# A two-layer feed-forward kernel with Winograd-style products: the next tile's x is split at the tile border, and one output block is carried in a PSUM bank

## The chip, the cores and the metric

The kernel runs on one core of a Trainium2 chip. The metric is the device time of one execution in microseconds (us). Before the change it is 1216.26 us, the median of three runs (1216.18 to 1216.88).

## The reference

An attention over 4 batches, 8 heads and 768 positions of width 64 (chunks of 32 queries that see 16 keys to the left, 8 to the right and 8 memory keys) gives a matrix of 3072 tokens by 512. Two feed-forward layers follow:

```
x = attention(q, k, v, mem_k, mem_v)            # 3072 x 512
h = x @ w_in;   g = where(h > 0, h, exp(min(h, 0)) - 1);   x = g @ w_out      # 512 -> 2048 -> 512
h = x @ w_in2;  g = s * max(h, 0)**2 + b;                  out = g @ w_out2   # 512 -> 2048 -> 512
```

All of it is float32. The kernel reaches the precision by writing every operand of a product as a high part and a low part.

## The kernel before, in words

**Tiles and products.** The 3072 tokens are cut into three tiles of 1024. Layer 0 takes them as tiles t=0, 1, 2, layer 1 as t=3, 4, 5 (the fourth to the sixth tile). A 2x2 block product is made with seven products instead of eight, in the order P1, P5, P6, P2, P7, P4, P3; blocks are called 11, 12, 21, 22. The sums of blocks that the products need are made beforehand: of x by GpSimd (`sums_of_x`, lines 806 to 816), of the weights by GpSimd (`prepare`), of g by VectorE (`sum_of`, line 1437).

**Steps.** TensorE's work is a list of 672 steps of six matmuls of 512 columns, 112 steps to a tile. Within a tile, s=0 to 27 is the up part of group 0 (two rounds of seven products by two steps), s=28 to 55 the down part of group 0 (seven products by four steps), s=56 to 69 and 70 to 83 the two up rounds of group 1, and s=84 to 111 the down part of group 1. A down product has four steps; x, the place within a down part, runs from 0 to 27, so that P1 is x=0 to 3, P7 x=16 to 19, P4 x=20 to 23, P3 x=24 to 27. `up` (line 989) multiplies with xc_hi and xc_lo, `down` (line 1004) with g_hi and g_lo. Steps and t count from 0.

**Banks.** Six accumulators of PSUM are in use: `acc_a` (P1, P2, P4), `acc_g` (P5, P3), `acc_e` (P6, P7), two banks each. `wait_bank` (line 958) is where TensorE waits for a bank: for P1 until the last block 21 is read out (`c21_done`), for P4 until block 11 is read out of `acc_a`. ScalarE seeds `acc_e` with P1's sum (`seed`, line 1132) and copies it out twice (`copy_s2`, line 1138, after P6; `copy_s3`, line 1144, after P7).

**The output y.** Group 0 writes the four blocks of y; group 1 adds to them. Block 21 in group 1 takes two additions of VectorE: `add_y21_u3` (after P7, at x=20 and 21) and `add_y21_p4` (after P4, at x=24 and 25), both by `add` (line 1354).

**Splits.** For each down step ScalarE makes g_hi (`cut_g`, line 1202) three steps ahead and VectorE g_lo (`lo_g`, line 1442) one iteration later; their ring has four places. For the next tile's x, ScalarE makes xc_hi (`split_x`, line 1122) and VectorE xc_lo (`lo_x`, line 1347) one iteration later: 14 pairs of 128x512 elements, one for each product and each kk in 0, 1. Which step makes which is the table `SPLIT_AT` for t=1 and 2 (it has kk=1 at s=107, 108, 110, 111, 113, 115 and 117) and `SPLIT_LATE` for t=3, 4, 5. The sums of x for kk=1 are made in place, so that GpSimd waits in `sums_of_x` until the low parts of P1 and later P2 are made.

**Weights.** GpSimd and ScalarE prepare the weights of both layers during the products: 7 pieces for each of 32 sets m. For a piece, ScalarE makes the high part (`cut_w`, line 1216) at the step that `hi_slot` names, GpSimd the low part (line 774), and SyncE's queue saves it to DRAM (line 617, 256 KB), from four places in turn (`wait_w_free`: a place is free when its save has landed). SyncE's queue also loads the weights of two steps at a time (line 636, 512 KB) into a ring of four. The 56 pieces of m=24 to 31 (layer 1, group 1) are made from t=2, s=94 on to t=3, s=70.

**Order.** There is no scheduler: ScalarE and VectorE each go through one loop over g, the number of the step, and emit in a fixed order within it what the tables place there. ScalarE: seeds and copies, then `relu` or `exp`, then `cut_g`, `split_x`, `cut_w`, then pieces of attention or copies of the output. VectorE: additions of the up part, P3's additions, `elu_of` or `square_of`, `sum_of`, `lo_g`, additions to y, `lo_x`, attention. GpSimd's order is written out at lines 834 to 858. In t=4 and 5 TensorE transposes the output of the tile before (`transpose_out`, line 955) ahead of every second step from s=2 to s=16; the first of them waits for both of P3's additions (`c12_done`).

Of the kernel before, what the change touches and what calls it, by code (L numbers as in the profile page):

```python
# [10 lines left out]
ACT = mybir.ActivationFunctionType  # L11
# [23 lines left out]
HALF = 512  # L35
TOK = 2 * HALF
TPL = NTOK // TOK
TILES = 2 * TPL
QUADS = 4
PHASE = 7 * QUADS  # L40
GROUP = 2 * PHASE
PER_TILE = 2 * GROUP
STEPS = PER_TILE * TILES
P1, P5, P6, P2, P7, P4, P3 = range(7)
X11, X12, X21, X22 = range(4)
# [120 lines left out]
def copies_before(r):  # L166
    return 2 * (r - r // 6)
# [36 lines left out]
def hi_slot(pp):  # L204

    if pp < PRODUCTS:
        return 4 + (pp - HEAD_PREP) * 11 // 10 + (3 if pp >= PREP_AT[PAIR + 1, P1] else 0)
    if pp < WIDE_END:
        return PER_TILE + 4 + (pp - PRODUCTS) * 3
    if pp < WIDE_END + 28:  # L210
        return 2 * PER_TILE + 2 + (pp - WIDE_END) * 5 // 2
    return 2 * PER_TILE + 94 + (pp - WIDE_END - 28) * 8 // 5


HI_SLOT = {pp: hi_slot(pp) for pp in range(HEAD_PREP, 2 * PRODUCTS)}
# [6 lines left out]
def saves_due(d):  # L222
# [6 lines left out]
HEAD_ORDER = [(c, pi) for c, pi, _ in HEAD_SPLITS]  # L229
SPLIT_AT = ((92, 93, 95, 96, 97, 98, 100), (107, 108, 110, 111, 113, 115, 117))  # L230
LOAD_AT = (88, 102)
SPLIT_LATE = ((P1, 0, 73), (P1, 1, 75), (P5, 0, 77), (P5, 1, 80), (P6, 0, 87), (P6, 1, 89), (P2, 0, 93), (P2, 1, 95),
              (P7, 0, 101), (P7, 1, 103), (P4, 0, 113), (P4, 1, 114), (P3, 0, 115), (P3, 1, 116))
LATE = [(pi, kk) for pi, kk, _ in SPLIT_LATE]
OUT_BLOCKS = TOK // 128
# [52 lines left out]
def build(nc, q, k, v, mem_k, mem_v, w_in0, w_out0, w_in1, w_out1, s_in, b_in, out):  # L288
# [8 lines left out]
    with ctx:  # L297
# [3 lines left out]
        def sem(name):  # L301
            return ctx.enter_context(nc.semaphore(name))
# [143 lines left out]
        c21_done = sem("c21_done")  # L446
        c12_done = sem("c12_done")
        y12_u2 = sem("y12_u2")
        y21_u3 = sem("y21_u3")
        y22_u3 = sem("y22_u3")  # L450
        y11_copied = sem("y11_copied")
        y11_added = sem("y11_added")
# [281 lines left out]
        def _(pool):  # L734
# [111 lines left out]
                sums_of_x(2, kk)  # L846
            for m in range(SETS + 4, SETS + 8):
                prepare((m,))
            for kk in range(2):
                sums_of_x(3, kk)  # L850
            for m in range(SETS + 8, 2 * SETS - 2):
                prepare((m,))
            sums_of_x(4, 0)
            for m in range(2 * SETS - 2, 2 * SETS):
                prepare((m,))
            sums_of_x(4, 1)
            for kk in range(2):
                sums_of_x(5, kk)

        @block.tensor  # L860
        def _(pe):
# [96 lines left out]
            def wait_bank(st, i):  # L958
                r = st.round
                if st.pi == P1 and r:  # L960
                    pe.wait_ge(c21_done, 2 * (r - 1) + i + 1)
                elif st.pi == P5 and r:
                    pe.wait_ge(c12_done, 2 * (r - 1) + i + 1)
                elif st.pi == P6:
                    pe.wait_ge(seeded, 2 * r + i + 1)
                elif st.pi == P7:
                    if r % 6 == 5:
                        pe.wait_ge(y12_u2, 2 * st.t + i + 1)
                    else:
                        pe.wait_ge(s2_done, copies_before(r) + i + 1)  # L970
                elif st.pi == P4:
                    wait_c11_read(pe, r, i)
                elif st.pi == P3:
                    pe.wait_ge(c22_done, 2 * r + i + 1)
# [20 lines left out]
            def down(st):  # L995
                k = split_of(st)
                pe.wait_ge(g_lo_done, k + 1)
                w = w_ring[:, st.g // 2 % W_RING, st.g % 2]
                for d in range(2):
                    if st.i == 0:  # L1000
                        wait_bank(st, d)
                    cols = slice(128 * d, 128 * d + 128)
                    for n, (a, x) in enumerate(((0, g_hi), (1, g_hi), (0, g_lo))):
                        last = nc.tensor.matmul(bank_of(st.pi, d), w[:, a, cols], x[:, k % RING, :],  # L1004
                                                start=(st.pi in (P1, P5, P4) and st.i == 0 and n == 0),
                                                stop=(st.i == QUADS - 1 and n == 2),
                                                skip_group_check=True)
                last.then_inc(step_done, 1)
# [61 lines left out]
        def _(act):  # L1070
# [53 lines left out]
            def seed(r, i, after):  # L1124
                act.wait_ge(step_done, after + 1)
                if r == 0:
                    act.wait_ge(e_cleared, i + 1)
                if r and r % 6 == 0:
                    act.wait_ge(y22_u3, 2 * (r // 6 - 1) + i + 1)
                elif r:  # L1130
                    act.wait_ge(s3_done, copies_before(r - 1) + i + 1)
                nc.scalar.activation(acc_e[i][:, :], acc_a[i][:, :], ACT.Copy).then_inc(seeded, 1)  # L1132

            def copy_s2(r, i, after):
# [11 lines left out]
            def copy_y11(p, d):  # L1146
                act.wait_ge(step_done, p.start + QUADS * P2 + QUADS)
                wait_y_free(act, p.t)
                nc.scalar.activation(y[:, d, 0:HALF], acc_a[d][:, :], ACT.Copy).then_inc(y11_copied, 1)

            def relu_of(d, pi, i):
                m = item_of(d.t, d.gr, 2 * d.u + i, pi)
# [90 lines left out]
            for g in range(STEPS + 2):  # L1243
# [10 lines left out]
                for p, x in downs_at(g):  # L1254
                    for d in range(2):
                        if x == 4 + d:
                            seed(p.round, d, p.start + QUADS * P1 + 3)
                        if x == 12 + d and p.gr == 0:
                            copy_s2(p.round, d, p.start + QUADS * P6 + 3)
                        if x == 16 + d and p.gr == 0:  # L1260
                            copy_y11(p, d)
                        if x == 20 + d and p.gr == 0:
                            copy_s3(p.round, d, p.start + QUADS * P7 + 3)
                for d, pi, i in items_at(g, 0):
                    if d.t >= TPL and pi == C11:
# [35 lines left out]
        def _(dve):  # L1301
# [48 lines left out]
            def y_at(b, d):  # L1350
                return y[:, d + 2 * (b // 2), HALF * (b % 2):HALF * (b % 2) + HALF]

            def add(to, a, b, done):
                nc.vector.tensor_tensor(to, a, b, ALU.add).then_inc(done, 1)  # L1354

            def make_c22(r, i, to, t=None):
                dve.wait_ge(s3_done, copies_before(r) + i + 1)
                if t is not None:
                    wait_y_free(dve, t)
                add(to, s3[:, i, :], acc_g[i][:, :], c22_done)  # L1360
# [22 lines left out]
                dve.wait_ge(y11_copied, 2 * p.t + d + 1)  # L1383
                add(y_at(X11, d), y_at(X11, d), acc_a[d][:, :], y11_added)

            def add_y21_u3(p, d):
                dve.wait_ge(step_done, p.start + QUADS * P7 + 4)
                dve.wait_ge(c21_done, 2 * (p.round - 3) + d + 1)
                add(y_at(X21, d), y_at(X21, d), acc_e[d][:, :], y21_u3)

            def add_y22_u3(p, d):
                dve.wait_ge(step_done, p.start + QUADS * P7 + 4)
                dve.wait_ge(c22_done, 2 * p.round + d + 1)
                add(y_at(X22, d), y_at(X22, d), acc_e[d][:, :], y22_u3)

            def add_y21_p4(p, d):
                dve.wait_ge(step_done, p.start + QUADS * P4 + 4)
                dve.wait_ge(y21_u3, 2 * p.t + d + 1)
                add(y_at(X21, d), y_at(X21, d), acc_a[d][:, :], c21_done)

            def add_y12_p3(p, d):
                dve.wait_ge(step_done, p.start + QUADS * P3 + 4)
# [64 lines left out]
            for g in range(STEPS + 2):  # L1467
# [26 lines left out]
                for p, x in downs_at(g):  # L1494
                    for d in range(2):
# [5 lines left out]
                        else:  # L1501
# [3 lines left out]
                                add_y12_u2(p, d)  # L1505
                            if x == 16 + d:
                                add_y11(p, d)
                            if x == 20 + d:
                                add_y21_u3(p, d)
                            if x == 22 + d:  # L1510
                                add_y22_u3(p, d)
                            if x == 24 + d:
                                add_y21_p4(p, d)
                for xt, kk, pi in x_split_at(g - 1):
                    lo_x(xt, kk, pi)
                for n, at in woven_at(g):
# [33 lines left out]
```

## Time and profile before

| | |
|---|---|
| median of 3 runs | 1216.26 us |
| profiled execution, its own time | 1211.64 us |
| its span, from the first to the last instruction | 1209.9 us |
| mean granted TensorE clock, as a share of full speed | 0.975 |
| busy: TensorE, VectorE, ScalarE, GpSimd | 1116.7, 845.4, 757.0, 425.8 us |
| attention before the first step, about | 120 us |
| bytes moved by DMA | 302.80 MB |

The profile names engines PE (TensorE's matmuls), PEld (its weight loads), DVE (VectorE), ACT (ScalarE), POOL (GpSimd) and SPq (SyncE's queue). A row of instructions has the source line, the engine, the operation, the tile written and the tiles read, the shapes and the count; behind the bar stand the busy time in us, the mean duration of one in ns, and the idle time of the engine ahead of them with what ended most of it. An instruction's duration reaches into the next one: VectorE's additions of 0.68 us start 0.60 us apart. Times of steps in the text are the starts of a step's first matmul.

### The profile page before, as it was taken

How to read it: one execution, taken by the hardware profiler on the slowest of the kernel's cores; microseconds unless marked ns; L12 is line 12 of the kernel's file. 1: busy time of each engine (PE TensorE's matmuls, PEld its weight loads, DVE VectorE, ACT ScalarE, POOL GpSimd, SP SyncE). 2: the span in 40 equal slices, each digit the busy share in tenths (PEclk: the TensorE clock that was granted, in tenths of full speed). 3: DMA queues.
4: the chain of work that ended last, by engine and by line, in shares of the span. 5: the costliest groups of instructions: out<-in, count | busy, mean ns of one | idle time of the engine just before them, and what ended most of it. 6: DMA issues, size and time to landing. Idle time of an engine off the chain costs nothing.

```text
span 1209.9 us, 18083 instructions
## 1 busy us (share of the span) xinstructions
PE 1116.7 (92%) x5787; PEld 880.7 (73%) x5787; DVE 845.4 (70%) x1246; ACT 757.0 (63%) x1775; POOL 425.8 (35%) x458
## 2 busy tenths in 40 slices
PE   8993998988899899989899898899999999999998
PEld 4662776766677778767687676677787887887876
DVE  5773478448966965896848966948938559567385
ACT  4864687567656857747647557657566476566463
POOL 5789369743231322134334265672001010000000
PEclk9986999999999999999999999999999999999999
DMA  9994999999788888859997599887587666786664
GB/s 213 270 270 150 292 334 312 315 306 301 228 280 219 257 248 262 265 188 349 303 288 226 165 352 396 299 311 231 177 233 259 196 193 175 198 225 189 192 189 157
DMA packets 203750, 302.80 MB, mean 250 GB/s; under 512 B 112520, under 2 KB 120712, under 8 KB 203656
## 3 DMA queue, kind: packets, MB, share of 16 engines
q1 hardware_dynamic: 203656, 301.65, 81.8%
q8 instruction: 47, 0.77, 0.2%
q14 instruction: 47, 0.39, 0.1%
HBM read 226.10 MB, written 75.50 MB: 249 GB/s over the span
## 4 chain that ended last, share of the span: by engine, by line
PE 55%; DVE 12%; DMA 6%; issue 5%; ACT 5%; POOL 4%; SPq 0%; ACTq 0%; DVEq 0%; POOLq 0%
PE ps L1004 28%; PE ps L989 23%; DMA w_ring<-w_scratch 3%; DVE g_lo L1442 2%; DVE X L1354 2%; ACT ps L1084 2%; DVE xc_lo L1347 1%; DVE T L1437 1%; DVE X L1437 1%; POOL w_new L774 1%; PE ps L903 1%; DVE X L1411 1%; PE ps L955 1%; POOL att L774 1%; ACT elu L1163 1%
## 5 line engine op out<-in xcount | busy, mean ns | idle before, releaser
L989 PE MATMUL ps<-xc_hi,w_ring 128*128 128x512 f32 x1344 | 438.3, 398 | 24.2 <-issue 9.8
L1004 PE MATMUL ps<-g_hi,w_ring 128*128 128x512 f32 x1344 | 423.6, 396 | 26.9 <-issue 15.9
L989 PEld LDWEIGHTS ps<-xc_hi,w_ring 128*128 128x128 f32 x1344 | 254.9, 190 | 84.0 <-issue 13.6
L1004 PEld LDWEIGHTS ps<-g_hi,w_ring 128*128 128x128 f32 x1344 | 248.2, 189 | 92.6 <-issue 28.2
L989 PE MATMUL ps<-xc_lo,w_ring 128*128 128x512 f32 x672 | 263.9, 393 | 0.0
L1004 PE MATMUL ps<-g_lo,w_ring 128*128 128x512 f32 x672 | 263.3, 392 | 0.0
L774 POOL TENSOR_TENSOR w_new<-w_raw,w_new 128x256 fp32r<-128x256 f32 x182 | 167.0, 921 | 207.6 <-ACT w_new L1216 204.2
L1442 DVE TENSOR_TENSOR g_lo<-X,g_hi 128x512 fp32r<-128x512 f32 x240 | 187.9, 789 | 45.5 <-ACT g_hi L1202 45.0
L1202 ACT ACTIVATE g_hi<-X 128x512 fp32r<-128x512 f32 x240 | 149.2, 628 | 80.2 <-PE ps L1004 76.8
L1354 DVE TENSOR_TENSOR X<-s,ps 128x512 f32<-128x512 f32 x144 | 96.3, 682 | 108.7 <-ACT s L1144 80.7
L1004 PEld LDWEIGHTS ps<-g_lo,w_ring 128*128 128x128 f32 x672 | 126.9, 189 | 27.5
L989 PEld LDWEIGHTS ps<-xc_lo,w_ring 128*128 128x128 f32 x672 | 127.7, 190 | 24.6
L1188 ACT ACTIVATE X<-X,sb_scalars 128x512 f32<-128x512 f32 x96 | 76.5, 809 | 34.2 <-DVE X L1417 34.1
L1084 ACT ACTIVATE ps<-ps,nbias 96x128 f32<-96x128 f32 x256 | 84.8, 332 | 8.5 <-DVE nbias L1310 8.4
L1442 DVE TENSOR_TENSOR g_lo<-T,g_hi 128x512 fp32r<-128x512 f32 x96 | 70.1, 750 | 20.7 <-ACT g_hi L1202 20.6
L1202 ACT ACTIVATE g_hi<-T 128x512 fp32r<-128x512 f32 x96 | 59.8, 629 | 39.0 <-PE ps L1004 38.6
L1216 ACT ACTIVATE w_new<-w_raw 128x256 fp32r<-128x256 f32 x140 | 57.3, 411 | 41.5 <-DMA w_scratch<-w_new 21.5
L1437 DVE TENSOR_TENSOR X<-X 128x512 f32<-128x512 f32 x96 | 75.6, 788 | 3.7 <-ACT X L1188 1.7
L1132 ACT ACTIVATE ps<-ps 128x512 f32<-128x512 f32 x72 | 41.6, 580 | 47.1 <-PE ps L989 46.1
L1354 DVE TENSOR_TENSOR y<-y,ps 128x512 f32<-128x512 f32 x84 | 56.7, 679 | 16.5 <-PE ps L1004 16.4
L1138 ACT ACTIVATE s<-ps 128x512 f32<-128x512 f32 x60 | 35.7, 597 | 48.8 <-PE ps L989 45.8
L774 POOL TENSOR_TENSOR att<-w_raw,att 128x256 fp32r<-128x256 f32 x42 | 40.8, 975 | 70.8 <-ACT att L1216 70.6
(115 smaller groups left out, 1343.2 us busy)
## 6 DMA issues: line engine op xcount, KB each, us to landing
w_ring<-w_scratch SPq DMA_DIRECT2D x336, 512.0 KB, 4.3
w_scratch<-w_new SPq DMA_DIRECT2D x182, 256.0 KB, 5.0
w_scratch<-att SPq DMA_DIRECT2D x42, 256.0 KB, 5.1
w_raw<-in_moe_w_in SPq DMA_DIRECT2D x16, 512.0 KB, 5.7
w_raw<-in_moe_w_out SPq DMA_DIRECT2D x16, 512.0 KB, 6.0
x_scratch<-y SPq DMA_DIRECT2D x3, 2048.0 KB, 9.8
att<-x_scratch SPq DMA_DIRECT2D x6, 1024.0 KB, 8.3
out<-elu SPq DMA_DIRECT2D x24, 256.0 KB, 4.4
```

Of the source, the lines that this page charges most:

```text
L774: nc.gpsimd.tensor_tensor(lo, src, hi.bitcast(F32), ALU.subtract).then_inc(w_lo_done, 1)
L989: last = nc.tensor.matmul(bank_of(st.pi, st.i), w[:, a, cols], x[:, st.pi, kk, :], start=(st.pi in (P1, P5, P4) and kk == 0 and n == 0), s ...
L1004: last = nc.tensor.matmul(bank_of(st.pi, d), w[:, a, cols], x[:, k % RING, :], start=(st.pi in (P1, P5, P4) and st.i == 0 and n == 0), sto ...
L1084: last = nc.scalar.activation(S_of(n)[:, h, :], S_of(n)[:, h, :], ACT.Exp, bias=nbias[:, i, h:h + 1], accum_out=rowsum[:, i, h, 0:1])
L1132: nc.scalar.activation(acc_e[i][:, :], acc_a[i][:, :], ACT.Copy).then_inc(seeded, 1)
L1138: nc.scalar.activation(s2[:, i, :], acc_e[i][:, :], ACT.Copy).then_inc(s2_done, 1)
L1188: nc.scalar.activation(h, h, ACT.Identity, scale=sb_scalars[:, 0:1], bias=sb_scalars[:, 1:2]).then_inc(affine_done, 1)
L1202: nc.scalar.activation(g_hi[:, k % RING, :], g_raw(st), ACT.Copy).then_inc(g_hi_done, 1)
L1216: nc.scalar.activation(w_at(pp)[:, 0].rearrange("p (c f) -> p c f", c=2), src, ACT.Copy).then_inc(w_hi_act, 1)
L1354: nc.vector.tensor_tensor(to, a, b, ALU.add).then_inc(done, 1)
L1437: nc.vector.tensor_tensor(to, a, b, ALU.subtract).then_inc(t_done, 1)
L1442: nc.vector.tensor_tensor(g_lo[:, k % RING, :], g_raw(st), g_hi[:, k % RING, :].bitcast(F32), ALU.subtract).then_inc(g_lo_done, 1)
```

## The change

It has three parts.

1. `SPLIT_LATE`: the 14 splits of x for t=3, 4, 5 stood at s=73 to 116, between other work. They now stand one at a step from s=106 of the tile before to s=7 of the tile itself (106 to 119), in the order P1, P2, P5, P6, P7, P4, P3 with kk=0 and 1 next to each other; the low part follows one step later. The old table is left under the name `LATE`, which the next line overwrites.
2. GpSimd's order and `hi_slot`: in t=2 the seven pieces of m=24 are prepared between `sums_of_x(3, 0)` and `sums_of_x(3, 1)` at unchanged steps (s=94 to 103). The 49 pieces of m=25 to 31 move from 1.6 steps apart from t=2, s=105 on, to 1.5 steps apart from t=3, s=2 to s=74. `sums_of_x(4, 0)` comes after the last weights, not between m=29 and m=30.
3. Block 21 of y in group 1: `seed_y21`, a copy of ScalarE, writes y21 of group 0 into P4's bank `acc_a` at x=17 and 18, once `add_y11` has read P2's sum from it. P4's first matmul no longer starts the accumulation and waits for `y21_seeded`. `copy_s3` now runs in group 1 too (x=20 and 21), and `make_y21` adds s3 and the bank into y at x=24 and 25. `add_y21_u3` and `add_y21_p4` go.

```diff
@@ hi_slot
-    return 2 * PER_TILE + 94 + (pp - WIDE_END - 28) * 8 // 5
+    if pp < WIDE_END + 35:
+        return 2 * PER_TILE + 94 + (pp - WIDE_END - 28) * 8 // 5
+    return 3 * PER_TILE + 2 + (pp - WIDE_END - 35) * 3 // 2
@@ tables
-SPLIT_LATE = ((P1, 0, 73), (P1, 1, 75), (P5, 0, 77), (P5, 1, 80), (P6, 0, 87), (P6, 1, 89), (P2, 0, 93), (P2, 1, 95),
+SPLIT_LATE = tuple((pi, kk, 106 + 2 * i + kk) for i, pi in enumerate((P1, P2, P5, P6, P7, P4, P3)) for kk in range(2))
+LATE = ((P1, 0, 73), (P1, 1, 75), (P5, 0, 77), (P5, 1, 80), (P6, 0, 87), (P6, 1, 89), (P2, 0, 93), (P2, 1, 95),
               (P7, 0, 101), (P7, 1, 103), (P4, 0, 113), (P4, 1, 114), (P3, 0, 115), (P3, 1, 116))
@@ gpsimd
-            for kk in range(2):
-                sums_of_x(3, kk)
-            for m in range(SETS + 8, 2 * SETS - 2):
+            sums_of_x(3, 0)
+            prepare((SETS + 8,))
+            sums_of_x(3, 1)
+            for m in range(SETS + 9, 2 * SETS):
                 prepare((m,))
-            sums_of_x(4, 0)
-            for m in range(2 * SETS - 2, 2 * SETS):
-                prepare((m,))
-            sums_of_x(4, 1)
-            for kk in range(2):
-                sums_of_x(5, kk)
+            for t in range(4, TILES):
+                for kk in range(2):
+                    sums_of_x(t, kk)
@@ tensor: wait_bank, down
+                elif st.pi == P4 and r % 6 == 5:
+                    pe.wait_ge(y21_seeded, 2 * st.t + i + 1)
-                                                start=(st.pi in (P1, P5, P4) and st.i == 0 and n == 0),
+                                                start=(st.pi in (P1, P5) + (P4,) * (1 - st.gr) and st.i == 0 and n == 0),
@@ scalar
+            def seed_y21(p, d):
+                act.wait_ge(y11_added, 2 * p.t + d + 1)
+                act.wait_ge(c21_done, 2 * (p.round - 3) + d + 1)
+                nc.scalar.activation(acc_a[d][:, :], y[:, d + 2, 0:HALF], ACT.Copy).then_inc(y21_seeded, 1)
-                        if x == 20 + d and p.gr == 0:
+                        if x == 17 + d and p.gr == 1:
+                            seed_y21(p, d)
+                        if x == 20 + d:
                             copy_s3(p.round, d, p.start + QUADS * P7 + 3)
@@ vector
-            def add_y21_u3(p, d):
-                dve.wait_ge(step_done, p.start + QUADS * P7 + 4)
-                dve.wait_ge(c21_done, 2 * (p.round - 3) + d + 1)
-                add(y_at(X21, d), y_at(X21, d), acc_e[d][:, :], y21_u3)
-            def add_y21_p4(p, d):
+            def make_y21(p, d):
                 dve.wait_ge(step_done, p.start + QUADS * P4 + 4)
-                dve.wait_ge(y21_u3, 2 * p.t + d + 1)
-                add(y_at(X21, d), y_at(X21, d), acc_a[d][:, :], c21_done)
+                dve.wait_ge(s3_done, 2 * p.round + d + 1)
+                add(y_at(X21, d), s3[:, d, :], acc_a[d][:, :], c21_done)
-                            if x == 20 + d:
-                                add_y21_u3(p, d)
...
-                                add_y21_p4(p, d)
+                                make_y21(p, d)
```

The counts of `s3_done` that `seed` and `make_c22` wait for change with it, from `copies_before(r)` to `2 * r`.

## Rows read from the trace of the kernel before

**Rows 1.** The page: busy time, share of the span and instructions of each engine.
```profile
PE 1116.7 (92%) x5787; PEld 880.7 (73%) x5787; DVE 845.4 (70%) x1246; ACT 757.0 (63%) x1775; POOL 425.8 (35%) x458
```
**Rows 2.** Chain that ended last, in time order: start us, us, what.
```profile
1007.06 1.36 issue
...
1045.12 0.44 PE ps L955 x4
...
1089.76 0.69 issue
...
1123.37 38.08 PE ps L989 x168
```
**Rows 3.** Windows: stretch, length, busy by engine (count), clock, DMA share, GB/s.
```profile
643.70:666.20 22.50, 19.54 (x85) 15.58 (x84) 21.32 (x26) 16.09 (x31) 12.26 (x8) 1.00 0.69 218
666.20:711.40 45.20, 40.17 (x170) 30.93 (x170) 40.91 (x61) 26.23 (x51) 21.31 (x21) 1.00 0.70 224
...
1084.20:1123.20 39.00, 38.31 (x169) 31.41 (x168) 28.70 (x46) 22.10 (x37) 0.00 (x0) 1.00 0.65 191
...
981.40:1000.50 19.10, 19.10 (x86) 15.71 (x85) 15.75 (x21) 14.80 (x26) 4.92 (x3) 1.00 0.65 192
838.60:880.40 41.80, 39.39 (x170) 31.16 (x169) 38.21 (x63) 22.47 (x37) 1.68 (x1) 1.00 0.60 176
1000.50:1042.20 41.70, 39.41 (x169) 31.12 (x168) 38.17 (x63) 22.48 (x37) 1.68 (x1) 1.00 0.61 176
711.40:756.60 45.20, 40.61 (x170) 32.43 (x169) 24.04 (x34) 28.69 (x57) 23.37 (x27) 0.96 1.01 384
756.60:799.50 42.90, 39.87 (x169) 30.97 (x168) 39.69 (x45) 27.18 (x53) 31.66 (x29) 1.00 0.85 286
```
**Rows 4.** Waits of PE from 643.7 to 666.2 us: total, times, longest.
```profile
PE ps L989 <- DVE X L1411: 3.0, 2, 2.4
```
**Rows 5.** Timeline around 695 us, ACT (t=2, s=99 to 102).
```profile
694.76 0.42 ACT L1216 ACTIVATE w_new<-w_raw 128x256 fp32r<-128x256 f32 x1 [6.59 <-POOL w_raw L788]
```
**Rows 6.** Timeline around 993 us, DVE and POOL (t=4, s=76 to 81).
```profile
990.98 1.61 POOL L806 TENSOR_TENSOR att<-att 128x512 f32<-128x512 f32 x1 [75.15 <-DVE xc_lo L1347]
...
993.06 1.78 DVE L1347 TENSOR_TENSOR xc_lo<-att,xc_hi 128x512 fp32r<-128x512 f32 x1
```
**Rows 7.** Timeline at the border of t=1 and t=2, DVE and POOL.
```profile
538.87 1.61 POOL L806 TENSOR_TENSOR elu<-elu 128x512 f32<-128x512 f32 x1 [13.91 <-DVE xc_lo L1347]
539.25 0.68 DVE L1354 TENSOR_TENSOR y<-y,ps 128x512 f32<-128x512 f32 x1
539.85 1.18 DVE L1347 TENSOR_TENSOR xc_lo<-elu,xc_hi 128x512 fp32r<-128x512 f32 x1
...
544.51 1.29 POOL L816 TENSOR_TENSOR elu<-elu 128x512 f32<-128x512 f32 x1 [0.63 <-DVE xc_lo L1347]
```
**Rows 8.** Timeline at the border of t=4 and t=5, ACT and DVE.
```profile
1034.27 0.64 ACT L1202 ACTIVATE g_hi<-X 128x512 fp32r<-128x512 f32 x1 [0.73 <-PE ps L1004]
...
1042.43 1.29 DVE L1354 TENSOR_TENSOR y<-y,ps 128x512 f32<-128x512 f32 x2 [3.48 <-PE ps L1004]
```
**Rows 9.** `cut_w` (L1216) from 711.4 to 799.5 us: count, durations, what it waited for.
```profile
L1216 ACT ACTIVATE w_new<-w_raw x33: 398/406/421, 713.9 to 795.1; 128x256 fp32r<-128x256 f32 x33
...
  DMA w_scratch<-w_new: 11.7, 7
```
**Rows 10.** The page: groups of copies of ACT and of additions of DVE.
```profile
L1132 ACT ACTIVATE ps<-ps 128x512 f32<-128x512 f32 x72 | 41.6, 580 | 47.1 <-PE ps L989 46.1
L1354 DVE TENSOR_TENSOR y<-y,ps 128x512 f32<-128x512 f32 x84 | 56.7, 679 | 16.5 <-PE ps L1004 16.4
L1138 ACT ACTIVATE s<-ps 128x512 f32<-128x512 f32 x60 | 35.7, 597 | 48.8 <-PE ps L989 45.8
```
**Rows 11.** Timeline around 1028 us, DVE and ACT (t=4, s=101 and 102).
```profile
1027.42 0.68 DVE L1354 TENSOR_TENSOR y<-y,ps 128x512 f32<-128x512 f32 x1
1027.45 0.63 ACT L1202 ACTIVATE g_hi<-T 128x512 fp32r<-128x512 f32 x1 [1.25 <-PE ps L1004]
```

More of the change, by code:

```diff
@@ L448, in build @@
         y12_u2 = sem("y12_u2")
-        y21_u3 = sem("y21_u3")
+        y21_seeded = sem("y21_seeded")
         y22_u3 = sem("y22_u3")
@@ L1130, in seed @@
                 elif r:
-                    act.wait_ge(s3_done, copies_before(r - 1) + i + 1)
+                    act.wait_ge(s3_done, 2 * (r - 1) + i + 1)
                 nc.scalar.activation(acc_e[i][:, :], acc_a[i][:, :], ACT.Copy).then_inc(seeded, 1)
@@ L1356, in make_c22 @@
             def make_c22(r, i, to, t=None):
-                dve.wait_ge(s3_done, copies_before(r) + i + 1)
+                dve.wait_ge(s3_done, 2 * r + i + 1)
                 if t is not None:
```

## The prediction

> **What bounds the kernel now.** I read the page first: TensorE is busy for 92% of the span, VectorE for 70%, ScalarE for 63% [rows 1]. So TensorE's own work is the floor, and what can be won is its idle time. The chain of waits says what a full pipe looks like: the 168 matmuls of the last up parts, 28 steps, take 38.08 us, which is 1.36 us a step [rows 2]. Against that I laid windows cut at the starts of the parts [rows 3]. A down part of layer 1 with no split of x in it and no weights being prepared takes 39.00 us (1084.2 to 1123.2), 0.92 over the floor. The two down parts of group 1 that hold splits of x take 41.80 (t=3) and 41.70 (t=4). In t=2 the second up round takes 22.50 against 19.10 for the same round of t=4, and the down part after it 45.20. In these stretches VectorE is the fullest engine behind TensorE: 38.2 of 41.7 and 40.9 of 45.2 us, against 28.7 in the clean part. Its late pieces end TensorE's waits: in t=2's up round, 3.0 us on the `elu_of` of L1411 [rows 4]; in t=4 a gap of 1.36 us in the chain, against 0.69 at the same place of the clean part [rows 2].
>
> In t=2 a second thing delays the down part. ScalarE stands for 6.59 us in a `cut_w` until GpSimd has made a sum of weights [rows 5]; GpSimd was itself waiting inside `sums_of_x(3, 1)`, ahead of the weights in its order. ScalarE is in order, so the `cut_g` behind it were late.
>
> **Part 1, the splits of x leave the busy stretch.** 14 pieces for each of three tiles leave s=73 to 116.
> - t=2, second up round: kk=1's sums on GpSimd and the low parts go; kk=0's sums stay. Taken at the clean round: 22.50 - 19.10 = 3.4 us gained.
> - t=2, down part: 45.20 against 39.00 is 6.2. Seven pieces of m=24 are still prepared there, and each GpSimd operation can hold a VectorE operation that reads two SBUF tiles (below). Of the 6.2, 2.7 is what the splits cost in t=4 (next item); the other 3.5 belong to ScalarE's wait and the weights, and of these I leave a good third, 1.3: 4.9 gained. Its ends: 2.7 (all 3.5 stay) and 6.2.
> - t=3 and t=4, down part: 41.80 - 39.00 and 41.70 - 39.00, 5.5 together. `sums_of_x(4, 0)` now falls in t=3 at s=76 to 82, so I take 0.5 off: 5.0 gained, between 4.0 and 5.5.
>
> Sum: 3.4 + 4.9 + 5.0 = 13.3 us gained.
>
> **Where they go: the border.** What must be ready when is the question, so I wrote VectorE's order out. Time 0 is the start of s=106. g_hi of s=109 is ready at about 0.8 (ScalarE's piece at 1034.27 begins 0.19 after that step's start and takes 0.64) [rows 8]. From there until the low part of P5, kk=1, VectorE does 13 operations: three `lo_g`, the second addition of y22, the two of y21, the first of P3, and six low parts of x (P1, P2, P5 by two). At 0.60 us from start to start that is 0.9 + 7.8 + 0.1 = 8.8. TensorE wants that piece at s=114, at 8 x 1.36 = 10.9. So without contention it is in time by 2.1 us.
>
> There is contention. `sums_of_x` for kk=1 starts once P1's low parts are made (4.6) and keeps GpSimd busy through three sums. The trace shows what that does: beside these sums a low part of x, with two SBUF tiles, takes up to 1.78 us instead of 0.68 [rows 6]. At the border of t=1 and t=2 the one begun at 539.85 took 1.18, while GpSimd's sum ran until 540.48; the addition from PSUM before it, inside the same sum, took 0.68 [rows 7]. Three low parts lie within the three sums: 3 x 1.10 = 3.3 more, so 12.1, and TensorE stalls 1.2 us at s=114. For t=4 and t=5 the output's transposes stand ahead of that step and wait for the second addition of P3, one operation further, 12.7: they could have gone at 10.9, so the stall is 1.8. P6's pieces, at 13.8, are wanted at 14.9 or later and cost nothing; what covers them is the stall before. Without the splits VectorE idles 3.48 us ahead of the border [rows 8]; that idle time is what the low parts use up.
>
> Cost: 1.2 + 1.8 + 1.8 = 4.8 us. From below 0: the border of t=1 and t=2 carries seven splits and the same sums. From above 9: each border 3.0, if the contention holds the three `lo_g` and P5's pieces too.
>
> The Trainium skill, SBUF — State Buffer, section "Who interferes with whom", speaks against this part of the change: a VectorE instruction with two SBUF inputs contends with GpSimd's reads, the lock is held for a whole instruction and the loser fully blocks, and one SBUF input does not contend. The rows above agree in kind. By that rule the worst case for each of the three pieces is a whole uncontended GpSimd sum, 1.29 us by the row at 544.51 [rows 7], instead of 1.10; the cost would be 0.6 us higher at each border.
>
> GpSimd is behind ScalarE's splits of P5, P6 and P4 for kk=1 as well. Its first sum ends at 6.3, before ScalarE's split of P5 at about 6.3 to 6.9; the third at 9.7, before P6's. ScalarE has nothing else there but its `cut_g` and the two seeds. Nothing added.
>
> **Part 2, the weights.** In t=2 ScalarE's 6.59 us wait goes, counted above. At the border no piece of weights is in flight any more. In t=3 the pieces come every 1.5 steps instead of 1.6, 49 of them after the border instead of 44. SyncE's queue has the same order of loads and saves; a save of 256 KB each moves later, none is added. The stretch is tight: the DMA share reads 1.01 in t=3's first up part and 0.85 in the down part behind it [rows 3], and `cut_w` waited 11.7 us in 7 times for a save to land [rows 9]. Demand rises by 1/15 for the weights alone; of the excess over the floor in these two parts, 45.2 + 42.9 - 2 x 38.08 = 11.9 us, I take an eighth, 1.5 us lost. Against it stands `sums_of_x(4, 0)`, which no longer cuts into the pieces of m=30 (0.9, the step at s=57 that came late). Net 0.6 lost, between 1.0 gained and 5 lost.
>
> **Part 3, y21 in the bank.** Off: 12 additions of 0.68 us (pitch 0.60) on VectorE, 7.2 us. On: 12 seeds of some 0.58 and 12 copies of 0.60 on ScalarE, 14.2 us [rows 10]. Both lie beside TensorE. The new wait is the seed's, for `add_y11`; behind it in ScalarE's queue stand the `cut_g` of s=104 and 105. In t=4 `add_y11` ran at 1027.42, just as ScalarE began that `cut_g` [rows 11], so it slips by 0.7 plus 0.6 to 1028.7, its low part is made by 1030.1, and TensorE wants it at 1031.36. The bank itself is ready at 1029.9. No stall in t=3 to 5; in t=0 to 2, where VectorE and ScalarE are both behind, two additions less may save a few tenths. I take 0.3 gained; the nearest rows bound it by 7.2 gained (all additions on the path) and 14.2 lost (all copies on it), and the clean part, which has no such wait, puts it near zero: 1.5 either way.
>
> **Sum:** 13.3 - 4.8 - 0.6 + 0.3 = 8.2 us less. The profiled execution took 1211.64 us (span 1209.9), 4.6 under the median of 1216.26. Its own forecast is 1203.4; against the median, **1208.1**.
>
> **The rivals.**
> - *The border is free* (0.20). For it: the border of t=1 and t=2 shows none of the wait with the same four sums. Against it: that one has half the low parts. Gain 8.2 + 4.8 = 13.0: 1203.3.
> - *The border takes more of it back* (0.16). Each border pays 3.0 instead of 1.6 on average: 8.2 - 4.2, so 4.0 gained: 1212.3. For it: VectorE's list there has no slack once it is late. Against it: TensorE's stall gives it time.
> - *Nothing comes out* (0.09). The stalls of the down parts are VectorE's own lateness from the up round, which the splits only share; they stay, and the border's cost eats what is left: 1216. The clean part, 2.7 us shorter with the same products, speaks against it. A slip in the tables, so that pieces are not where the diff says, would look the same.
> - *The saves set the pace in t=3* (0.09), the slower side. 33 pieces took 88.1 us there, 2.67 us each [rows 3, 9]. If the landing of saves through four places is what paced them, then 56 steps with a piece every 1.5 steps, 37.3 pieces, take 37.3 x 2.67 = 99.6 us: 11.5 lost, net 3.3 slower: 1219.6. It decides from the point where more than about two thirds of that pacing holds. Against it: in the second stretch the DMA share is 0.85, and ScalarE waited for saves in only 7 of 33 pieces.
>
> **Chances and range.** Forecast 0.46, the rivals 0.20, 0.16, 0.09 and 0.09. About 0.2% (2.4 us) is what a measurement of this kernel can tell from no change. Faster by more: the forecast and the first two rivals, 0.82, less 0.02 for the low ends of the gains, 0.80. Within: 0.11, the third rival and those 0.02. Slower: 0.09, the last. The range takes in the free border, 1203.3, with 0.8 for the other unknowns, and the dear border, 1212.3, with 2.7 for t=2's down part and the weights at their bad ends: 1202.5 to 1215, the last two rivals outside.
>
> **What would show it.** Right: t=2's second up round near 19.1 and its down part near 40.3; t=3's and t=4's down parts near 39.2; no wait of ScalarE for L788; a stall of 1 to 2 us at s=114 in each of three borders, ended by the low part of P5 or P3's addition, with low parts of 1.2 to 1.8 us beside GpSimd's sums. Wrong: no stall there, or stalls at s=114 and s=116 of 3 us; the down parts unchanged; or t=3's first two parts longer than 91 us together, with `cut_w` waiting far over 12 us for saves.

## The result and the profile after

The changed kernel takes 1200.78 us, the median of four runs (1200.37 to 1206.85), against 1216.22 for the kernel before in the same job. The ratio of the runs is 0.9895, with a 95% interval of 0.9872 to 0.9918, which is 12.8 us off 1216.2 (10.0 to 15.6); the medians themselves lie 15.4 apart. In the next job it was 0.9897 (0.9875 to 0.9920), with medians of 1199.51 and 1212.29. So it is faster, as forecast. The size was short: 8.2 us were forecast, and the median of 1200.78 lies 1.7 us below the lower end of the range; 0.9895 of 1216.26 would be 1203.5, inside it.

The kernel before scatters more than its first three runs showed: its medians in the later jobs were 1212.3, 1213.7, 1213.5 and 1212.3 us, with single runs from 1209 to 1219 (two runs of 1550 us in one job are left aside). Times a few us apart can't be told from each other by runs alone. The traces can do more: without attention and without weights in preparation, a part of layer 1 has the same length to 0.05 us in two traces of the same kernel, apart from t=4's first up part (44.37 and 44.19 in the changed kernel).

The windows of the changed kernel, cut at the same steps as [rows 3] (columns as there): t=2's second up round and last down part, t=3's first up and first down part, t=3's and t=4's last down parts, t=5's first up part.

```profile
643.00:662.10 19.10, 19.10 (x86) 15.80 (x85) 17.67 (x23) 14.47 (x28) 8.53 (x6) 1.00 0.80 253
662.10:701.00 38.90, 38.27 (x169) 31.42 (x168) 37.56 (x56) 27.22 (x51) 15.71 (x12) 1.00 0.80 248
701.00:744.40 43.40, 39.03 (x170) 31.28 (x169) 28.84 (x38) 29.66 (x59) 25.61 (x29) 1.00 0.98 364
744.40:790.20 45.80, 42.21 (x169) 33.18 (x168) 41.69 (x48) 28.73 (x58) 32.42 (x32) 0.93 0.88 302
828.60:868.70 40.10, 38.70 (x170) 31.39 (x169) 36.58 (x58) 25.35 (x42) 3.42 (x3) 1.00 0.63 182
990.20:1029.20 39.00, 38.31 (x169) 31.43 (x168) 35.46 (x56) 25.33 (x42) 3.36 (x3) 1.00 0.66 189
1029.20:1072.90 43.70, 42.14 (x202) 34.59 (x201) 26.11 (x40) 29.33 (x50) 3.12 (x2) 1.00 0.77 216
```

Line by line against [rows 3]: 22.50 became 19.10; 45.20 became 38.90; 45.20 and 42.90 (the weights' stretch) became 43.40 and 45.80; 41.80 became 40.10; 41.70 became 39.00. The last line is the price: the same part of the kernel before took 42.0 us. ScalarE's wait of [rows 5] is down to 1.0 us, from the groups of instructions of t=2's last down part:

```profile
L1224 ACT ACTIVATE w_new<-w_raw 128x256 fp32r<-128x256 f32 x7 | 2.8, 404 | 1.0 <-POOL w_raw L791 1.0
```

The border of t=4 and t=5, in the timeline of VectorE and GpSimd. L1357 is `lo_x`, L1364 the helper of all additions, L809 to L819 the four sums of x:

```profile
1025.77 1.61 POOL L809 TENSOR_TENSOR att<-att 128x512 f32<-128x512 f32 x1 [120.06 <-DVE xc_lo L1357]
1026.14 0.68 DVE L1364 TENSOR_TENSOR y<-s,ps 128x512 f32<-128x512 f32 x1
1026.74 4.58 DVE L1357 TENSOR_TENSOR xc_lo<-att,xc_hi 128x512 fp32r<-128x512 f32 x3
1027.46 1.62 POOL L811 TENSOR_TENSOR att<-att 128x512 f32<-128x512 f32 x1
1029.04 1.73 POOL L815 TENSOR_TENSOR att<-att 128x512 f32<-128x512 f32 x1
1030.91 1.55 POOL L819 TENSOR_TENSOR att<-att 128x512 f32<-128x512 f32 x1
1031.24 0.68 DVE L1364 TENSOR_TENSOR y<-y,ps 128x512 f32<-128x512 f32 x1
1031.84 1.17 DVE L1357 TENSOR_TENSOR xc_lo<-att,xc_hi 128x512 fp32r<-128x512 f32 x1
1032.94 0.68 DVE L1364 TENSOR_TENSOR y<-y,ps 128x512 f32<-128x512 f32 x1
```

Three low parts take 4.58 us beside GpSimd's first three sums. P3's first addition, which could have begun when t=4's last step ended (1029.4), begins at 1031.24; between it and the second stands a low part of P5. The low parts follow each other 1.11, 1.70 and 1.69 us apart and leave VectorE no idle time, so they wait for no split of ScalarE. TensorE's waits tell who held it, first in t=5's first up part, then in t=3's:

```profile
PE ps L956 <- DVE y L1364: 1.6, 1, 1.6
```
```profile
PE ps L992 <- DMA w_ring<-w_scratch: 3.1, 2, 2.0
PE ps L992 <- DVE xc_lo L1357: 1.3, 1, 1.3
```

Into t=5 it is the transposes (L956) that wait for P3's second addition; into t=3 it is the low part of P5 itself.

### The profile page after: what moved, and what is told of

The parts are those of the page before. It is cut to its first block and busy times, and to the rows that moved or that the text cites. A ratio compares the mean times of both kernels' runs of the same rounds, so it can differ in the third digit from the quotient of the medians.

```text
span 1198.7 us, 18107 instructions
## 1 busy us (share of the span) xinstructions
PE 1112.6 (93%) x5787; PEld 883.2 (74%) x5787; DVE 844.5 (70%) x1234; ACT 769.0 (64%) x1799; POOL 426.8 (36%) x458
## 5 line engine op out<-in xcount | busy, mean ns | idle before, releaser
L1007 PEld LDWEIGHTS ps<-g_hi,w_ring 128*128 128x128 f32 x1344 | 251.1, 190 | 79.9 <-issue 19.6
L1364 DVE TENSOR_TENSOR X<-s,ps 128x512 f32<-128x512 f32 x144 | 96.3, 682 | 93.2 <-ACT s L1147 62.8
L809 POOL TENSOR_TENSOR att<-att 128x512 f32<-128x512 f32 x6 | 9.6, 1602 | 194.7 <-DVE xc_lo L1357 166.9
```

## The experiments

Twelve more kernels ran. I compare parts of their traces, in us, between the starts of the same steps.

**The same kernels again.** No edit.

> The changed kernel once more, for its time beside the others and for a second trace. Expected 1200.8 us, within 1.5; the three stalls at the tile borders (start of s=1 to start of s=2 in t=3, 4, 5) 2.8, 3.5 and 3.5 us long as in its first trace, and t=0 to the first half of t=2, where the change does little, differing by some tenths from trace to trace.

> The kernel before once more, for a second trace. Theory: t=2's second up round 22 to 23 us and its down part 44 to 45, t=3's and t=4's down parts 41.7 as in its first trace; what differs between traces lies in t=0, t=1 and the first two parts of t=3, where attention and the saves of weights are in the DMA queues. Rival: one of the gains read from the first pair of traces is chance, and its part moves by over 1 us.

The changed kernel took 1199.51 us (four runs), the kernel before 1212.73 (one run). Most parts from t=2's last down part on repeat: the three borders within 0.01, t=2's last down part 38.96 and 38.97, t=4's last 39.05 and 39.05; of the kernel before t=3's last down part 41.75 and 41.73, t=4's 41.76 and 41.75. The kernel before's t=2 repeats to 0.7 (22.57 and 23.25; 45.13 and 44.76). What moves is attention ahead of the first step (120.4 and 116.8 in the changed kernel), t=0 and t=1, by up to 2.8 in one part, and t=3's first two parts: 88.1 and 90.6 together in the kernel before, 89.2 and 89.6 after. So I also compare the whole stretch from t=2, s=70 to the end of the span: 566.2 and 568.9 in the kernel before, 555.6 and 555.9 after, 10.6 less in the first pair and 13.0 in the second. t=2's second up round and t=3's first two parts in the kernel before's second trace:

```profile
642.10:665.30 23.20, 20.79 (x85) 16.85 (x84) 21.82 (x26) 16.48 (x32) 12.26 (x8) 0.93 0.65 210
...
710.10:757.10 47.00, 40.85 (x169) 32.37 (x168) 23.30 (x32) 28.26 (x56) 23.05 (x26) 0.96 0.99 371
757.10:800.70 43.60, 39.93 (x170) 30.99 (x168) 40.43 (x47) 27.29 (x53) 32.43 (x29) 1.00 0.84 282
```

**Part 3 alone, and all without part 3.** The first is the kernel before with the third part of the diff; the second the changed kernel with `add_y21_u3` and `add_y21_p4` as before.

> The kernel before with part 3 alone (y21 in the bank). Theory: 12 additions less on VectorE and 24 copies more on ScalarE all lie beside TensorE; 0 us against the kernel before, within 1.5, and the down parts of t=3 and t=4 stay at 41.8 and 41.7 us. Rival: the additions lay on the path where VectorE was late (t=2 to 4, s=99 to 105), and the part alone gives 3 us or more; then those down parts fall under 41.2.

> The changed kernel without part 3: splits and weights as after the change, y21 with two additions of VectorE. Theory: within 1.5 us of the changed kernel, the stalls at the border as long as there (1.4, 1.8, 1.8 us over the step without one). Rival: the two additions at x=20 and 21 push VectorE's list at the border by 1.2 us, and each of the three stalls grows by up to 1.2, 3.6 us in all.

Part 3 alone: 1213.02 us, ratio 0.9999 (0.9982 to 1.0016); the down parts of t=3 and t=4 stay at 41.70 and 41.80. Without it: 1201.66 us, ratio 0.9913 (0.9889 to 0.9938), and every part of t=3 to t=5 within some 0.3 of the changed kernel, apart from the first two of t=3, which scatter. VectorE is busy 36.79 us in t=4's last down part without it and 35.46 with it, ScalarE 23.28 and 25.33, at the same 39.00 us:

```profile
989.80:1028.80 39.00, 38.31 (x169) 31.42 (x168) 36.79 (x58) 23.28 (x38) 3.36 (x3) 1.00 0.64 190
```

The stalls at the border don't grow. Beside the splits at the border part 3 moves work and no time. Alone it moves none that the runs can tell (2 us either way), but its trace shows where it helps: in t=2's last down part, where VectorE is late, s=104 to 107 took 5.54 us together against 6.35 to 6.38 in three traces without it (the two of the kernel before and that of part 2 alone). The part took 43.96 for their 44.8 to 45.2:

```profile
665.80:709.80 44.00, 39.80 (x170) 31.02 (x169) 38.97 (x59) 27.06 (x53) 19.61 (x19) 1.00 0.68 211
```

In the changed kernel these four steps take 5.44 with part 3 and without it, so nothing is left there for it to give.

**What the border's stall is made of.** GpSimd's late sums for kk=1 made on 16 columns; the other 496 columns of these sums are left out:

```diff
                 late = t >= TPL
+                if late and kk:
+                    x11, x12, x21, x22, t1, t2, t4 = (b[:, 0:16] for b in (x11, x12, x21, x22, t1, t2, t4))
```

> The changed kernel, with the four sums of x on GpSimd for kk=1 in t=3, 4, 5 made on 16 of 512 columns (the other 496 columns of those sums are left out). Theory: the stall at the border comes from VectorE's low parts that wait for GpSimd's sums; with sums of a thirtieth of the length the low parts take 0.68 us, the low part of P5 is ready 2 us ahead, and the three stalls (1.4, 1.8 and 1.8 us) go to 0 to 0.3 each: 4 to 5 us under the changed kernel. Rival: the number of pieces is what makes VectorE late; at least 1 us of each stall stays, and the kernel gains under 2 us.

All three stalls went to 0: the first step pair of t=3, t=4 and t=5 is 1.42, 1.78 and 1.77 us shorter, 4.97 in all, and t=5's first up part 41.92 for 43.67. The timeline of VectorE and GpSimd at the border of t=4 and t=5:

```profile
1027.15 0.54 POOL L811 TENSOR_TENSOR att<-att 128x16 f32<-128x16 f32 x1 [118.61 <-DVE xc_lo L1359]
...
1028.12 1.89 DVE L1359 TENSOR_TENSOR xc_lo<-att,xc_hi 128x512 fp32r<-128x512 f32 x3
1029.48 0.60 POOL L821 TENSOR_TENSOR att<-att 128x16 f32<-128x16 f32 x1 [1.32 <-DVE xc_lo L1359]
1030.80 0.69 DVE L1366 TENSOR_TENSOR y<-y,ps 128x512 f32<-128x512 f32 x1 [0.80 <-PE ps L1009]
```

The same three low parts take 1.89 us for 4.58, and VectorE waits 0.80 for TensorE ahead of P3's addition. The fourth, P5's for kk=1, takes 0.69 for 1.17. So the pieces alone fit ahead of the border and cause no stall; the 3.2 us of contention on top of them do. The whole kernel took 1198.75 us, ratio 0.9886 (0.9861 to 0.9910), 0.8 to 2.0 under the changed kernel's medians and not the 4 to 5 expected, a difference that the runs can't tell from the scatter; from t=2, s=70 to the end its trace is 2.7 to 3.0 shorter. t=5's first up part kept its gain whole, t=3's first two parts (89.8) show none.

**Which piece TensorE waits for.** P5 ahead of P2 in the new table, nothing else:

```diff
-... enumerate((P1, P2, P5, P6, P7, P4, P3)) ...
+... enumerate((P1, P5, P2, P6, P7, P4, P3)) ...
```

> The changed kernel with P5's splits ahead of P2's in the new table (P1, P5, P2, ...), P3's additions left where they are. Theory: the low part of P5 is ready 1.5 us or more ahead of its step. At the border into t=3, where no output is transposed, the stall falls from 1.4 to 0.5 or less; into t=4 and t=5 TensorE still waits for P3's second addition before the transposes, and 1.2 us or more of the 1.8 stay. Rival: all three stalls are the low part of P5, and all three go.

As the theory had it: into t=3 the step from s=1 to s=2 falls from 2.78 to 1.72, into t=4 and t=5 only from 3.50 to 3.00, still behind P3's second addition, in the waits of t=5:

```profile
PE ps L956 <- DVE y L1364: 1.1, 1, 1.1
```

But in t=3 the step at s=3 takes 0.8 more (2.16 for 1.38), so that most of what P5 gave back there is lost two steps on. Its one run took 1203.44 us.

**A border without the stall.** TensorE's own order, and both of P3's additions in the first iteration of the new tile:

```diff
+SPLIT_LATE = tuple((pi, kk, at + kk) for pi, at in ((P1, 106), (P5, 108), (P6, 111), (P2, 113), (P7, 115), (P4, 117), (P3, 119))
+                   for kk in range(2))
...
-                        if x == PHASE + d and p.gr == 1:
+                        if x == PHASE and p.gr == 1:
                             add_y12_p3(p, d)
```

> The changed kernel with another border: splits in the order in which TensorE needs them (P1 at s=106, P5 at 108, P6 at 111, P2 at 113, P7 at 115, P4 at 117, P3 at 119), and both of P3's additions to y at once, one step earlier for the second. Theory: the low parts of P5 now run under GpSimd's first two sums, and P3's additions come right behind them, at about 1.6 us after the border, ahead of TensorE's need at 2.7; all three stalls (1.4, 1.8, 1.8 us) go to 0 to 0.3, and the kernel is 4 to 5 us under the changed one. Rival: GpSimd's sums hold VectorE whatever the order, so the stall moves to P6 or P2 (s=4 or s=6) and at least half of it stays.

The stalls at s=1 are gone, all three (1.36, 1.72 and 1.72 us, the plain step and the step with transposes), and nothing comes back at s=3 or s=5: t=4's and t=5's first up parts are 1.87 and 1.75 shorter (t=3's, 45.41 against 43.35 and 45.15 in the changed kernel's two traces, scatters by more than the stall). The timeline of VectorE shows P3's two additions at 1025.38, 0.3 after the border at 1025.1, between P5's low parts and P6's:

```profile
1022.57 1.19 DVE L1356 TENSOR_TENSOR xc_lo<-att,xc_hi 128x512 fp32r<-128x512 f32 x1
...
1023.96 1.50 DVE L1356 TENSOR_TENSOR xc_lo<-att,xc_hi 128x512 fp32r<-128x512 f32 x1 [0.20 <-ACT xc_hi L1124]
...
1025.38 1.27 DVE L1363 TENSOR_TENSOR y<-y,ps 128x512 f32<-128x512 f32 x2
1026.58 1.48 DVE L1356 TENSOR_TENSOR xc_lo<-att,xc_hi 128x512 fp32r<-128x512 f32 x2
```

It took 1198.1 us (1194.44 to 1200.11, six runs), ratio 0.9869 (0.9844 to 0.9894): 1.4 to 2.7 under the changed kernel's medians, where 4 to 5 were expected, and not told apart by the runs. From t=2, s=70 to the end its trace is 2.3 to 2.5 shorter, although it has 0.8 more in t=2's second up round, by a wait for a load of weights that the other traces of the new table don't show. The contention at the border is still there, in 1.19 and 1.50 for 0.68, but TensorE doesn't wait for it any more. That both edits are needed at the borders of t=4 and t=5 rests on `order_only`; the earlier addition alone was not tried.

**Part 2 alone.** The kernel before with the new `hi_slot` and the sums for t=4 behind the last weights.

> The kernel before with part 2 alone, as far as it can stand alone: the 49 pieces of m=25 to 31 every 1.5 steps from t=3, s=2 on, and the sums for t=4 behind the last weights; the seven pieces of m=24 stay behind the sums for t=3. Theory: t=2 keeps its stalls (22.5 and about 44 us), t=3's first two parts stay within 1.5 us of the 88 to 91 us of the traces with the old pace, t=3 s=57 loses its stall of 0.9: within 3 us of the kernel before. Rival: the saves set the pace, and t=3's first two parts take 95 us or more.

1215.91 us, ratio 1.0021 (1.0004 to 1.0037). t=3's first two parts took 90.0, within the 88 to 91 of the old pace, and the 1.0 at s=57 went. But it lost 6.3 us that I hadn't foreseen, in t=3's second up round (25.36 for 19.07): the sums for t=4 now ran for both kk from s=76 on, seven in a row, beside the splits of P1 and P5 at s=73 to 80 and the sums of g. TensorE's waits in that round:

```profile
PE ps L989 <- DVE X L1354: 3.6, 1, 3.6
```

So part 2 loses without part 1. With the splits at the border only the four sums for kk=0 run there, as those for kk=1 wait for P1's low parts, and they cost 1.3 (below). Part 1 can't stand without part 2's order: with the splits at the border and the sums for t=3 left ahead of the weights of m=24, ScalarE would wait for a sum of weights that GpSimd makes only after ScalarE's own later split, and neither would go on.

**ScalarE's wait in t=2.** The kernel before with P2 and P6 exchanged in the old table (s=87, 89 and 93, 95), so that GpSimd's sums end before m=24 is due.

> The kernel before with P2's and P6's splits exchanged in the old table (P2 at s=87 and 89, P6 at 93 and 95): as many pieces at the same steps, but GpSimd's last sum of x for t=3 no longer waits for s=96, so that the weights of m=24 are in time and ScalarE does not stand for 6.6 us. Theory: in t=2's down part the wait for the weights is worth about 3.5 us and the splits 2.7; the part falls from 45.1 to 41 to 42, and t=3's and t=4's down parts stay within 0.5 us of 41.7. Rival: the pieces of x themselves hold that part up, and it stays above 44.

The wait for L788 fell from 6.6 to 1.9 us:

```profile
ACT w_new L1216 <- POOL w_raw L788: 1.9, 1, 1.9
```

The part fell to 42.89, short of the 41 to 42 expected. The four late steps at s=99, 100, 101 and 104 gave back 3.9 us, s=87 another 1.0 (0.6 against the second trace), but with the sum that was moved s=95 and 96 take 2.0 more, and s=111 took 1.0 more, a wait for a load of weights. t=3 and t=4 stayed at 41.75. So ScalarE's wait is a cause of its own, of some 3.9 of the part's 6.2; the rest goes only with the splits. That the moved sum is what holds VectorE at s=95 is argued from its place, not shown by a kernel. Its one run took 1212.27 us.

**The pace of the weights.** Every 1.75 steps for 1.5: `* 7 // 4` for `* 3 // 2` in `hi_slot`.

> The changed kernel with the 49 pieces every 1.75 steps instead of 1.5 (the last one at s=86 instead of s=74). Theory: t=3's first two parts are held up by the DMA queues there, which carry a seventh less for weights; they get 1 to 3 us shorter than the 89.2 and 89.6 us of the changed kernel, and the next parts of t=3 lose some of it, as pieces of weights now meet them. Rival: what holds those two parts up is VectorE and the loads of x and y, not the pace of the weights, and they stay within 0.5 us.

t=3's first two parts took 86.0, 3.2 under the changed kernel's first trace and 3.6 under its second; `cut_w` waited for saves for 4.9 us for 9.8. But t=3's last down part grew from 40.09 to 44.55, more than expected. The sums for t=4, behind the last weights, now fell into it at s=89 to 91, as the timeline of GpSimd shows (the first two of four):

```profile
833.21 1.73 POOL L809 TENSOR_TENSOR att<-att 128x512 f32<-128x512 f32 x1
835.01 1.61 POOL L811 TENSOR_TENSOR att<-att 128x512 f32<-128x512 f32 x1
```

1203.85 us, ratio 0.9922 (0.9900 to 0.9945): a gain given back. The next kernels tell how much of it is the sums (2.6) and how much the pieces of weights (2.9).

**Both, with the sums put elsewhere.** `border_new` with the pace of 1.75 and `sums_of_x(4, 0)` ahead of m=30 again; and `border_new` with the sums alone moved so.

```diff
-            for m in range(SETS + 9, 2 * SETS):
+            for m in range(SETS + 9, 2 * SETS - 2):
                 prepare((m,))
-            for t in range(4, TILES):
+            sums_of_x(4, 0)
+            for m in range(2 * SETS - 2, 2 * SETS):
+                prepare((m,))
+            sums_of_x(4, 1)
...
```

> The border as in border_new, with a piece of weights every 1.75 steps and the sums for t=4 ahead of the last two sets of weights (about s=61 of t=3), not behind them. Theory: t=3's first two parts as with the pace of 1.75 alone (86 us) less the border's 1.4, its later parts within 1 us of the changed kernel's (78.4), so that 3 to 4 us come on top of border_new's 4.9: 7 to 9 us under the changed kernel. Rival: the pieces of weights that now reach into t=3's last down part (to s=86) hold up VectorE there and cost 2 us or more.

> border_new, its pace of 1.5 steps kept, with the sums of x for t=4, kk=0, ahead of the last two sets of weights again (about s=53 of t=3), as in the kernel before. Theory: the 1.0 us by which t=3's last down part (40.1) exceeds t=4's (39.05) is these sums at s=76 to 82; it goes to 39.1 to 39.3, and the step at s=57 takes 0.9 us more again, as in the kernel before: no change in sum, within 0.5 us over these two places. Rival: the 1.0 us comes from the weights that now run until s=74, and the part stays at 40.

The first took 1195.22 us (1194.28 to 1199.57, six runs), ratio 0.9866 (0.9841 to 0.9892). t=3's first two parts took 86.8, 2.8 under `border_new`'s 89.7, and its last down part 41.9 for 40.1, 1.8 given back, because pieces of weights reach into it: the gain is 1 us and not 3 to 4. Against the 44.55 of the slower pace with the sums in the same part, the sums' place is worth 2.6. The second took 1197.48 us, ratio 0.9882 (0.9862 to 0.9903); t=3's last down part went from 40.10 to 39.06, as expected, as the sums now ran at 789 to 794 us with VectorE hardly busy, 1.29 each. Against this kernel's 39.06, the pieces of weights in `border_pace` cost 2.9. The second up round ahead of it took 19.04 for 19.35. The 0.9 at s=57 did not come back, against the expectation (1.36 us there). The last down part:

```profile
829.50:868.60 39.10, 38.41 (x170) 31.45 (x169) 35.36 (x56) 24.30 (x40) 3.38 (x3) 1.00 0.65 190
```

By the ratios these three and the changed kernel can't be ordered (0.9895, 0.9869, 0.9866, 0.9882, each with some 0.0025 either way); by the traces the three border steps are 5.0 us shorter together in each of the three. All of them beat the kernel before, and by the traces the changed one: from t=2, s=70 to the end `border_new` takes 553.3 us, `border_pace` 551.3 and `border_sums` 553.3, the changed kernel 555.6 and 555.9.

## Why the prediction was right, and where it was not

The terms, in us, forecast and as the first pair of traces has them:

| term | forecast | traces |
|---|---|---|
| t=2, second up round | -3.4 | -3.5 |
| t=2, last down part | -4.9 | -6.2 |
| t=3 and t=4, last down parts | -5.0 | -4.4 |
| three borders | +1.2, +1.8, +1.8 | +1.4, +1.8, +1.8 |
| t=3, first two parts without the border's stall | +1.5 | -0.4 |
| t=3, s=57, and the next round | -0.9 | -0.8 |
| y21 | -0.3 | 0 |
| sum | -8.2 | -10.3 |

The second pair of traces would give -4.2, -5.8, -4.3, the same +5.0, -2.5, -0.7 and 0: -12.5. What differs is t=3's first two parts and the kernel before's t=2.

- **The border** was the step that carried most risk, and it held: the contention with GpSimd's sums, the stalls of 1.2 to 1.8 us, and that P3's second addition, not P5's low part, ends the wait where the output is transposed. Written out, VectorE's order gave P3's second addition at 12.7 us after the start of s=106; in the trace its end is 1033.62, 12.56 after 1021.06. Part of the closeness is luck: three pieces with 1.10 each were put in, 3.3, and four were held, by 0.5, 1.1, 1.1 and 0.5, 3.2 in all. `small_sums` and `border_new` show cause and cure, `order_only` the place.
- **t=2's down part** is the first mis-sized term. "I leave 1.3 of it" for the weights of m=24 was wrong: beside them the part takes 38.96, as one without weights. With the splits gone VectorE is busy for 37.56 of 38.90 us there, and the part is still only 0.9 over 28 plain steps, as the clean part of layer 1 is.
- **The weights' pace**: "I take an eighth, 1.5 us lost" found nothing that shows. Less the border's stall, t=3's first two parts took 87.8 to 91.3 us in eight traces with the new pace (the changed kernel 87.8 and 88.1, `no_y21` 88.6, part 2 alone 90.0, `small_sums` 89.8, `order_only` 90.6, `border_new` 89.7, `border_sums` 91.3), and 88.1, 90.6, 91.3 and 88.4 in four with the old one (the third with part 3 alone, the fourth `p2_early`). The two sets overlap: a loss or gain of a us can't be told, and the table's -0.4 is one draw from this scatter. The slower rival, 11.5 us, is refuted for this pace; that the stretch does depend on the pace is shown the other way: with 1.75 steps it took 84.6 less the stall, and 86.8 in `border_pace`, below all twelve.
- **The sums for t=4** in t=3: 0.5 was taken; `border_sums` shows 1.04, and 0.3 in the round before.
- **y21**: right for the reason given, and the few tenths put on t=2 are there in the old surrounding (0.8). The seed that could have held up `cut_g` waited 3.7 us in two of its twelve calls, and no part of layer 1 got longer.
- **The level.** I took the gain off a median of 1216.26 that later jobs put at 1212 to 1214, and the changed kernel came out at 1199.5 to 1200.8. By the first pair of traces the terms make 2.1 us more than forecast (10.3 for 8.2): t=2's down part 1.3 and t=3's first two parts 1.9 more, the others together 1.1 less. The ratio's 12.8 is above that too. The second pair makes 12.5, most of the difference in t=3's first two parts, where the first trace of the kernel before was at the short end. Whole, from t=2, s=70 to the end, the pairs show 10.6 and 13.0 less, and the ratio's 12.8 lies between them. How much of the medians' 15.4 is t=0 and t=1, which the change hardly touches and which move by 2 to 3 us from trace to trace, stays open.

The Trainium skill, SBUF — State Buffer, "SBUF: two separate sides" and "Who interferes with whom", was weighed at 0.6 us more a border for a lock over a whole instruction. The border into t=3 cost 0.2 more than forecast, the others nothing. In kind the traces agree: the low part of [rows 7] begun at 539.85 ended at 541.03, 0.55 after GpSimd's sum (538.87 to 540.48) was through, and VectorE's additions with one operand in PSUM took 0.67 to 0.69 in all 252 cases of the changed kernel's trace.

## What to carry to other kernels

Write out the order of the in-order engine around the new place of the work, with the pitch and the contended durations of its own trace, and ask of each operation who waits for it: here that gave three stalls to within 0.2 us, and later the order that removes them. When work moves to a new place, put there what TensorE waits for next (here P3's additions) ahead of what is only due later. And compare parts of traces before whole times, when the whole scatters by more than the change is worth.

## What the runs showed of the hardware that was not expected

**A wait of some 3 us can cost more than itself.** After TensorE's step at t=3, s=31, which took 4.22 us in the changed kernel, the granted clock fell to 0.50 of full speed, which is the lower of its two levels, 1.2 GHz, and the next steps took 2.25, 2.73 and 2.56 us for 1.36, windows of 3 us:

```profile
747.00:750.00 3.00, 3.00 (x15) 2.49 (x14) 3.00 (x5) 1.36 (x3) 1.48 (x2) 1.00 0.85 338
750.00:753.00 3.00, 0.51 (x3) 0.08 (x1) 2.72 (x5) 2.62 (x5) 0.26 (x1) 1.00 0.84 266
753.00:756.00 3.00, 2.17 (x7) 1.55 (x8) 2.76 (x4) 3.00 (x8) 2.98 (x3) 0.79 0.48 127
756.00:759.00 3.00, 3.00 (x8) 2.30 (x7) 3.00 (x4) 1.91 (x4) 2.86 (x3) 0.50 0.59 223
759.00:762.00 3.00, 3.00 (x9) 2.37 (x8) 3.00 (x5) 0.99 (x3) 0.41 (x2) 0.58 0.78 218
762.00:765.00 3.00, 3.00 (x14) 2.45 (x14) 3.00 (x4) 1.57 (x3) 2.92 (x3) 1.00 1.04 375
```

TensorE had been busy for 0.51 of 3 us in the window before the fall. The shares of 0.79, 0.50 and 0.58 in the three windows from 753 on make 6.8 us at the lower level, most of them with TensorE busy all the time, before full clock came back. The lower clock is part of the 45.80 us of that down part (mean clock 0.93), and of `weights_only`'s loss, where a step of 5.14 us was followed by 2.70 and 2.56. The border's stalls, with a gap of 1.3 to 1.6 us, left the clock alone. A longer one doesn't always lower it: t=2's s=79 took 3.92 and 3.93 us in the two traces of the kernel before, with the same wait of 2.4 us, and the mean clock of that round was 1.00 in the first [rows 3] and 0.93 in the second; the step behind took 2.18 and 2.70 and the next 1.50 and 1.66. That is the 0.7 by which the round's two traces differ.

**GpSimd loses too, though less.** Its sum of 128x512 takes 1.29 us where no low part runs and 1.54 to 1.74 beside the low parts, 0.2 to 0.5 more; VectorE's low part goes from 0.68 to up to 1.78. With 16 columns GpSimd's sum takes 0.22 to 0.60.
